# Attention, experts and FFN on one core: how the bias stage feeds the first head pair

## What is computed

```
scores = scale * np.matmul(q, k.transpose(0, 1, 3, 2))
psi_rel = np.log1p(np.abs(rel))
psi_i = np.log1p(np.maximum(pos[:, None].astype(np.float32), 1.0))
x = (psi_rel / psi_i)[..., None]
h = np.maximum(x @ w1 + b1, 0.0)
bias = h @ w2
scores = scores + bias.transpose(2, 0, 1)[None, :, :, :]
```

## Time and profile before

| | us |
|---|---|
| median of 3 runs | 1107.94 |
| lowest and highest | 1107.51, 1108.87 |
| profiled execution, its own time | 1108.25 |
| its span in the profile | 1106.4 |
| bias stage in it: first hidden tile to last store issued | 8.3 to 64.4 |
| TensorE busy over the span | 1060.3 (96%) |
| VectorE busy | 742.5 (67%) |
| ScalarE busy | 484.6 (44%) |
| GpSimd busy | 202.9 (18%) |

### The profile page before, as it was taken

One profiled execution on the slowest core, in us unless ns is written; L12 is line 12 of the kernel. 1 busy time (PEld: TensorE's weight loads), 2 busy tenths in 40 slices (PEclk: granted clock), 3 DMA queues, 4 the chain that ended last, 5 costly groups with the idle time before them and its releaser, 6 DMA issues.

```text
span 1106.4 us, 23091 instructions
## 1 busy us (share of the span) xinstructions
PE 1060.3 (96%) x7160; PEld 937.0 (85%) x7161; DVE 742.5 (67%) x1249; ACT 484.6 (44%) x972; POOL 202.9 (18%) x196
## 2 busy tenths in 40 slices
PE   5889999999999989999999999999999999999996
PEld 2367777777776889999999989999999999999995
DVE  8965555565655745775646479977777777777764
ACT  6987767677776343654444243221211212112111
POOL 2035525252540231221212000010010100100101
PEclk9999999999999989999999999999999999999998
DMA  4973643735531581773523180020000100100000
GB/s 138 293 227 83 179 111 84 204 82 118 168 69 33 176 292 52 201 201 50 201 50 88 59 257 1 22 58 0 28 28 0 57 0 0 57 0 0 29 1 29
DMA packets 87126, 103.11 MB, mean 93 GB/s; under 512 B 49536, under 2 KB 60800, under 8 KB 87088
## 3 DMA queue, kind: packets, MB, share of 16 engines
q1 hardware_dynamic: 83056, 89.27, 28.9%
q0 software_dynamic: 4032, 13.37, 4.3%
HBM read 77.25 MB, written 25.37 MB: 93 GB/s over the span
## 4 chain that ended last, share of the span: by engine, by line
PE 86%; DVE 5%; issue 3%; DMA 2%; ACT 2%; POOL 1%; SPq 0%; DVEq 0%; ACTq 0%; POOLq 0%
PE psum L1721 25%; PE psum L1737 12%; PE psum L1237 10%; PE psum L1246 10%; PE psum L443 8%; PE psum L562 7%; PE psum L547 6%; PE psum L267 3%; PE psum L575 2%; DVE f_eg L1676 1%; PE psum L1223 1%; DMA bias_ihj<-b_res 1%; DMA f_vraw<-fv 1%; ACT a_pr L672 0%; PE psum L1282 0%
## 5 line engine op out<-in xcount | busy, mean ns | idle before, releaser
L1676 DVE RECIPROCAL f_eg<-f_eg 128x384 f32<-128x384 f32 x72 | 183.2, 2545 | 0.0
L1643 ACT ACTIVATE f_eg<-psum 128x384 f32<-128x384 f32 x72 | 35.4, 492 | 330.9 <-PE psum L1721 330.9
L611 DVE CUSTOM_DVE_ANT_0 a_sc<-psum,a_bias 128x576 f32<-128x576 f32 x144 | 108.1, 753 | 79.9 <-PE psum L443 60.2
L1721 PE MATMUL psum<-f_x,f_ghi 128*128 (+1 forms) x576 | 147.8, 337 | 2.3 <-DVE f_eg L1680 1.1
L1721 PE MATMUL psum<-f_x,f_vhi 128*128 (+1 forms) x576 | 146.1, 334 | 0.0
L672 ACT ACTIVATE a_pr<-a_sc,a_nmax 128x576 f32<-128x576 f32 x144 | 111.6, 775 | 39.3 <-DVE a_nmax L611 32.8
L1721 PEld LDWEIGHTS psum<-f_x,f_ghi 128*128 128x128 f32 x576 | 105.7, 188 | 9.2 <-issue 2.6
L547 PE MATMUL psum<-ident,a_pr 128*128 128x128 f32 x720 | 102.5, 273 | 2.3 <-ACT a_pr L672 1.6
L1721 PEld LDWEIGHTS psum<-f_x,f_vhi 128*128 128x128 f32 x576 | 104.0, 188 | 0.0
L443 PE MATMUL psum<-a_khi,a_qs 128*128 128x288 f32 x320 | 102.5, 337 | 1.0 <-DVE a_nmax L611 0.7
L1611 POOL DMA_INDIRECT out<-f_ob,f_cols x18 | 17.5, 974 | 466.8 <-ACT f_ob L1629 463.5
(11 more groups left out here) (240 smaller groups left out, 2355.8 us busy)
## 6 DMA issues: line engine op xcount, KB each, us to landing
e_raw<-ew SPq DMA_DIRECT2D x16, 1024.0 KB, 9.7
bias_ihj<-b_res SPq DMA_DIRECT2D x36, 288.0 KB, 2.8
a_qraw<-q SPq DMA_DIRECT2D x32, 288.0 KB, 5.3
a_kraw<-k SPq DMA_DIRECT2D x32, 288.0 KB, 5.8
a_bias<-bias_ihj SPq DMA_DIRECT2D x16, 576.0 KB, 6.9
xn_t<-e_yn SPq DMA_DIRECT2D x8, 576.0 KB
a_v<-v SPq DMA_DIRECT2D x32, 128.0 KB, 2.4
x_tokens<-a_xp SPq DMA_DIRECT2D x64, 64.0 KB, 1.7
```

The lines of the kernel that those rows point to most:

```text
L611: e.tensor_tensor_reduce(sc[:, h, :].rearrange("p (a s) -> p a s", a=2), s_ps[:, h, :, 0:HALF], bias[:, 2 * s + h, :].rearrange("p (c s) - ...
L1643: e.activation(self.eg[:, k % 2, :], self.g_ps[k % 2][:, 0:CHUNK], ACT.Exp, scale=-1.0).then_inc(self.s_e, 1)
L1676: e.reciprocal(x, x).then_inc(self.s_c, 1)
L1721: mm = e.matmul(acc[:, 0:CHUNK], a, b, start=(q == 0 and i == 0), stop=(q == KD - 1 and i == 2))
```

## The change

Bias tiles are loaded one head at a time, in 288 KB with packets of 2304 bytes, after steps 11, 12, 19, 20, 27, 28 and, for the fourth tile, behind the store of step 35. v of the first pair is loaded after steps 13 to 16, q and k of the second pair in four transfers after steps 21 to 24, the gate weights after steps 0 and 1. In the later pairs a bias tile is also loaded as two transfers. GpSimd no longer casts the first pair; VectorE does, behind its last hidden tile: cast and subtraction of k, eviction of step 33, cast and subtraction of q, eviction of step 35. ScalarE leaves these two evictions out and loads the exponential's table behind the eviction of step 34. TensorE and the stores wait for VectorE's evictions by a semaphore of their own.

```diff
@@ -107,7 +107,8 @@
     CT = S + OFF
     CUT = 508
     PER = NS // 4
-    TILES = {10: 0, 18: 1, 26: 2, 34: 3}
+    TILES = {11: (0, 0), 12: (0, 1), 19: (1, 0), 20: (1, 1), 27: (2, 0), 28: (2, 1), 35: (3, 0)}
+    SHARED = (NS - 3, NS - 1)
     place = arena.run(arena.FRONT)
     table = place("b_table", [P, CT])
     dist_i = place("b_dist_i", [P, CT], i32)
@@ -131,7 +132,7 @@
     upper, lower = slice(CUT, CT), slice(0, CUT)
     s_id, s_z, s_w, s_io, s_go, s_d, s_ln, s_tab, s_low = (
         sem("b_" + n) for n in ("id", "z", "w", "io", "go", "d", "ln", "tab", "low"))
-    s_hp, s_hv, s_mm, s_ev = sem("b_hp"), sem("b_hv"), sem.loop("b_mm"), sem.loop("b_ev")
+    s_hp, s_hv, s_mm, s_ev, s_evd = sem("b_hp"), sem("b_hv"), sem.loop("b_mm"), sem.loop("b_ev"), sem("b_evd")
     s_st = [sem.loop(f"b_st{u}") for u in range(4)]
 
     def hidden(e, s, par, r4, done):
@@ -146,8 +147,10 @@
 
         def store(it, u):
             s = it * 4 + u
-            e.wait_ge(s_ev, sem.at(s_ev, s + 1))
-            sem.apart(e, s + 1)
+            if s in SHARED:
+                e.wait_ge(s_evd, sem.at(s_evd, SHARED.index(s) + 1))
+            else:
+                e.wait_ge(s_ev, sem.at(s_ev, s + 1 - sum(x < s for x in SHARED)))
             e.dma_start(biasd[bass.ds(s * P, P), :], res[:, u, :]).then_inc(s_st[u], 16)
 
         def landed(steps):
@@ -156,11 +159,14 @@
         for s in range(NS):
             store(s // 4, s % 4)
             if s in TILES:
-                landed(8 * TILES[s] + 8)
-                more["bias tile"](e, TILES[s])
+                t, h = TILES[s]
+                if h == 0:
+                    landed(8 * t + 8)
+                more["bias tile"](e, t, (h,))
             more["loads"](e, s)
+        more["bias tile"](e, 3, (1,))
         landed(NS)
-        more["bias tile"](e, 4)
+        more["bias tile"](e, 4, (0, 1))
 
     def gpsimd(e):
         e.memset(warm[:, :], 0.0).then_inc(s_z, 1)
@@ -216,7 +222,16 @@
         with e.Fori(1, PER) as it:
             for u in range(4):
                 step(it, u)
-        more["VectorE"](e)
+
+        def evict(s):
+            u = s % 4
+            e.wait_ge(s_mm, sem.at(s_mm, s + 1))
+            e.wait_ge(s_st[u], sem.at(s_st[u], s // 4 * 16))
+            e.tensor_scalar(res[:, u, :].rearrange("p (a b) -> p a b", a=2), acc[:, u, :, 0:HALF],
+                            invp[:, s:s + 1], None, ALU.mult).then_inc(s_evd, 1)
+        for i, s in enumerate(SHARED):
+            more["VectorE"](e, i)
+            evict(s)
 
     def scalar(e):
         e.wait_ge(s_z, sem.at(s_z, 1))
@@ -239,6 +254,8 @@
             e.wait_ge(s_mm, sem.at(s_mm, s))
             if following:
                 hidden0(s + 3, (u + 3) % 4)
+            if not following and s in SHARED:
+                return
             e.wait_ge(s_mm, sem.at(s_mm, s + 1))
             e.wait_ge(s_st[u], sem.at(s_st[u], it * 16))
             e.activation(res[:, u, :].rearrange("p (a b) -> p a b", a=2), acc[:, u, :, 0:HALF], ACT.Copy,
@@ -250,9 +267,8 @@
             for u in range(4):
                 step(it, u, True)
         for u in range(4):
-            if u == 3:
-                more["ScalarE"](e)
             step(PER - 1, u, u == 0)
+        more["ScalarE"](e)
 
     def tensor(e):
         e.wait_ge(s_w, sem.at(s_w, 16))
@@ -267,9 +283,10 @@
                         mm = e.matmul(acc[32 * r4:32 * r4 + 32, u, half, 0:HALF], w2d,
                                       hid[:, u, r4, half * HALF:(half + 1) * HALF], start=True, stop=True)
                 mm.then_inc(s_mm, 1)
-        for h in range(2):
-            e.wait_ge(s_ev, sem.at(s_ev, NS - 3 + h))
-            more["TensorE"](e, h)
+        e.wait_ge(s_ev, sem.at(s_ev, NS - 3))
+        more["TensorE"](e, 0)
+        e.wait_ge(s_evd, sem.at(s_evd, 1))
+        more["TensorE"](e, 1)
     return sync, tensor, scalar, vector, gpsimd
 
 
@@ -310,12 +327,18 @@
         sem.loop("a_" + n) for n in ("s", "b", "e", "t", "o", "oe", "bk", "r", "x"))
     s_kept = [sem.loop(f"a_t{g}") for g in range(3)]
 
-    def load_qk(e, pair, u, halves=(0, 1)):
-        for half in (slice(64 * i, 64 * i + 64) for i in halves):
+    def load_half(e, pair, u, i, of_k):
+        half = slice(64 * i, 64 * i + 64)
+        if of_k:
+            e.dma_start(kraw[half, u, :], kt[bass.ds(pair, 1), :, :].rearrange("a p s -> p (a s)")).then_inc(s_k[u], 16)
+        else:
             e.dma_start(qraw[half, u, :, :].rearrange("p a s -> p (a s)"),
                         qt[bass.ds(pair, 1), :, :, :].rearrange("a p h s -> p (a h s)")).then_inc(s_q[u], 16)
-            e.dma_start(kraw[half, u, :], kt[bass.ds(pair, 1), :, :].rearrange("a p s -> p (a s)"))\
-                .then_inc(s_k[u], 16)
+
+    def load_qk(e, pair, u):
+        for i in range(2):
+            for of_k in range(2):
+                load_half(e, pair, u, i, of_k)
 
     def load_v(e, pair, u, parts=range(4)):
         va, vb = (v[bass.ds(pair % B * H + pair // B * 2 + h, 1), :, :] for h in range(2))
@@ -326,14 +349,16 @@
         for i in parts:
             e.dma_start(*cuts[i]).then_inc(s_v[u], 16)
 
-    def load_bias(e, hp, s):
+    def load_bias(e, hp, s, heads=(0, 1)):
 
         if s == MIX:
-            for a in range(2):
+            for a in heads:
                 e.dma_start(bias[64 * a:64 * a + 64, 2 * s, :], biasd[BLK:S, bass.ds(hp * 2 + a, 1), :]
                             .rearrange("i a j -> i (a j)")).then_inc(s_bias[s], 16)
         else:
-            e.dma_start(bias[:, 2 * s:2 * s + 2, :], biasd[s * P:s * P + P, bass.ds(hp * 2, 2), :]).then_inc(s_bias[s], 16)
+            for h in heads:
+                e.dma_start(bias[:, 2 * s + h, :], biasd[s * P:s * P + P, bass.ds(hp * 2 + h, 1), :]
+                            .rearrange("i a j -> i (a j)")).then_inc(s_bias[s], 16)
 
     def set_constants(e):
         for u in range(2):
@@ -344,18 +369,21 @@
             e.tensor_copy(xw[:, :, h, 0:64], ident[:, 64 * h:64 * h + 64].unsqueeze(1).to_broadcast([P, H // 2, 64]))\
                 .then_inc(s_init, 1)
         e.wait_ge(s_init, sem.at(s_init, 5))
+
+    def first_split(e, part):
+
+        if part:
+            low = both(0, slice(64, P))
+            e.wait_ge(s_q[0], sem.at(s_q[0], 32))
+            e.wait_ge(s_init, sem.at(s_init, 2))
+            e.tensor_copy(both(0, slice(0, P)), qraw[:, 0, :, :]).then_inc(s_qh, 1)
+            e.wait_ge(s_qh, sem.at(s_qh, 1))
+            e.tensor_tensor(low, qraw[64:P, 0, :, :], low.bitcast(f32), ALU.subtract).then_inc(s_low, 1)
+            return
         e.wait_ge(s_k[0], sem.at(s_k[0], 32))
         e.tensor_copy(khi[:, 0, :], kraw[:, 0, :]).then_inc(s_sp, 1)
-        e.wait_ge(s_q[0], sem.at(s_q[0], 32))
-        e.tensor_copy(both(0, slice(0, P)), qraw[:, 0, :, :]).then_inc(s_qh, 1)
-
-    def first_low(e):
-
-        low = both(0, slice(64, P))
         e.wait_ge(s_sp, sem.at(s_sp, 1))
         e.tensor_tensor(klo[:, 0, :], kraw[:, 0, :], khi[:, 0, :].bitcast(f32), ALU.subtract).then_inc(s_low, 1)
-        e.wait_ge(s_qh, sem.at(s_qh, 1))
-        e.tensor_tensor(low, qraw[64:P, 0, :, :], low.bitcast(f32), ALU.subtract).then_inc(s_low, 1)
 
     def split_k(e, it, u):
 
@@ -391,17 +419,17 @@
 
     def loads(e, step):
 
+        if step in (0, 1):
+            if step == 0:
+                e.wait_ge(s_init, sem.at(s_init, 3))
+            e.dma_start(xw[64 * step:64 * step + 64, :, step, 64:XW],
+                        wg.rearrange("(p h d) e -> h d p e", h=2, d=64)[step]).then_inc(s_wg, 16)
         if step in (2, 4, 6, 8):
             small(e, step // 2 - 1)
-        if step in (12, 14, 16, 20):
-            if step == 12:
-                e.wait_ge(s_init, sem.at(s_init, 3))
-            load_v(e, 0, 0, ((12, 14, 16, 20).index(step),))
-        if step in (22, 24):
-            load_qk(e, 1, 1, (step // 2 - 11,))
-        if step in (28, 30):
-            h = step // 2 - 14
-            e.dma_start(xw[64 * h:64 * h + 64, :, h, 64:XW], wg.rearrange("(p h d) e -> h d p e", h=2, d=64)[h]).then_inc(s_wg, 16)
+        if step in (13, 14, 15, 16):
+            load_v(e, 0, 0, (step - 13,))
+        if step in (21, 22, 23, 24):
+            load_half(e, 1, 1, (step - 21) // 2, (step - 21) % 2)
 
     def split_done(e, p):
 
@@ -606,7 +634,7 @@
             unit = p * TPP + 2 * s + h
             e.wait_ge(s_s, sem.at(s_s, unit + 1))
             e.wait_ge(s_e, sem.at(s_e, unit if s == 0 and h == 0 else unit - 2 if s == 0 else unit - 1))
-            e.wait_ge(s_bias[s], sem.at(s_bias[s], (p // B + 1) * (32 if s == MIX else 16)))
+            e.wait_ge(s_bias[s], sem.at(s_bias[s], (p // B + 1) * 32))
             sem.apart(e, p)
             e.tensor_tensor_reduce(sc[:, h, :].rearrange("p (a s) -> p a s", a=2), s_ps[:, h, :, 0:HALF],
                                    bias[:, 2 * s + h, :].rearrange("p (c s) -> p c s", c=2),
@@ -724,7 +752,7 @@
 
```

(2 more changed lines are left out.)

## The result

The changed kernel takes 1109.78 us (median of 20 runs, 1107.45 to 1112.36) where the kernel before takes 1107.47 in the same comparison (20 runs, 1105.81 to 1111.34): ratio 1.0021, 95% interval 1.0013 to 1.0028. The forecast was 1106.4, range 1105.0 to 1108.7. The profiled execution has an own time of 1110.77 us and a span of 1108.9, against 1108.25 and 1106.4.

A forecast was written before the change was run, and what follows sets the result against it. TensorE holds 86% of the chain, so only an earlier start of the first pair, where ScalarE is late, was to count: 1108.25 - 1.5 = 1106.75, less 0.3 as that execution lay above the median, 1106.4; range 1105.0 to 1108.7.

The forecast's parts named there:

- GpSimd's casts go: Bias stage: without GpSimd's casts VectorE's hidden tiles aren't stretched, and the last ends 1.78 us earlier, at 55.43.
- What VectorE gets in their place: VectorE behind its last hidden tile: two casts at 0.87 us, two subtractions, two evictions at 0.75, ending at 61.11.
- The eviction of step 33 waits for a store: VectorE's eviction of step 33 waits for step 29's store, landing at 57.7, and starts at 57.8: costs 0.3 us.
- rival D: First pair: all cover holds, no store wait and a short cast; gain 1.8 to 2.0 us, 1105.7; chance 0.13.
- Rival A: VectorE's casts run at one column a cycle, 1.36 us instead of 0.87; costs 1.0 us, 1107.4; chance 0.10.
- B: Step 33's eviction waits for a store landing at 59.9; first exponential at 64.7, 0.75 us slower, 1108.7; chance 0.12.
- The gain at the first exponential: ScalarE's first exponential of the first pair comes at 62.47 instead of 63.96 us, a gain of 1.5 us.
- Moves that cost nothing: Moved loads and extra transfers, also in later pairs, are covered; SyncE pays some 0.4 us each, no tile is late.
- All later stages hang on the first pair and shift with it: Behind the first pair: every later stage moves earlier by the same 1.5 us gained at the first exponential.
- Rival C: First pair's start isn't what binds; later tiles or next pairs' v and q take the gain back, 1107.9; chance 0.10.
- slower: Whole kernel measured above 1110.2 us, from the tail of the case where step 33's eviction waits long; chance 0.04.

The follow-up runs named there:

- engines_only: Kernel before with only the casts and two evictions moved to VectorE and the table load behind step 34's eviction; loads as before: ratio 1.0002.
- loads_only: Kernel before with only the loads spread and cut by head; casts stay on GpSimd, evictions on ScalarE: ratio 1.0019.
- before_own_tokens: Kernel before with the experts' token-list stores on a semaphore of their own: ratio 1.0005 to the kernel before.
- before_plus_16: Kernel before plus 16 small loads that nothing reads, issued by SyncE near 103 us: ratio 1.0030.
- before_own_tokens_2: Repeat on another chip of the kernel before with the token-list stores on their own semaphore: ratio 1.0021.
- after_whole_own_tokens: Changed kernel with the later pairs' bias tiles whole again and the token-list stores on their own semaphore: ratio 1.0007 to the kernel before.

## Why the prediction was wrong

**"GpSimd's casts go": right.** No hidden tile is stretched any more (0.52 to 0.55 us each); the last ends at 55.45, forecast 55.43.

**"What VectorE gets in their place": right, with the cast a little dear.** 0.79 and 0.75 us where 0.87 was taken. The estimate of 0.76 worked out from the Trainium skill's page (VectorE: DVE Perf Modes, The perf-mode tier table) agrees with the second. The eviction from PSUM took 0.81 and 0.82 instead of 0.75.

**"The eviction of step 33 waits for a store": right in kind, too small.** In the first profile of the changed kernel it started at 57.43, at once, as in rival D, and the first exponential stood at 62.24, forecast 62.5. That was luck: the other six changed fronts waited 0.35 to 1.22 us, so the wait is 0.7 in the mean of seven where 0.3 was taken. Rival A is out, and so is B's wait of 2.5 us.

**The gain at the first exponential: 0.5 us in the mean, where 1.5 was forecast.** The first two profiles differ by 1.72, but the earlier trace rows has the exponential 0.2 later than the mean of its kernel, and the changed one's first profile has it 1.0 earlier than the mean of its own. And what is gained doesn't outlast the pair. TensorE's pause before the first scores, 2.3 to 3.4 us in the seven changed fronts, and the half clock behind it were not in the working. From the first transposes to the routing's first matmul an unchanged front takes 299.6 us (ten of eleven profiles), a changed one 299.9 to 300.7. engines_only, which has the row of work on VectorE but not the spread loads, has a pause of 1.56 us, full clock and 299.6; loads_only has half clock and 300.4. So this loss comes with the loads' part, and not with the row on VectorE alone. At the routing the changed front stands at 364.70 in the mean of seven, the unchanged one at 364.30 in the mean of eleven: the front's gain is nil or a small loss.

**The step that failed for the sign** is in "Moves that cost nothing": "In later pairs four extra transfers in each of three reloads cost SyncE some 0.4 us each; a tile has 1 us and more to spare". That priced the transfers by the engine that issues them and by the tile that waits. Both were right: no later tile was late. But together with the four of the first pair they changed when other transfers of the same queue land, 580 us on, at a place that has no slack: TensorE's pause there was 0.51 us already, and 0.38 us stays when nothing waits for the lists (before_own_tokens). The price, by the first two profiles, is 2.7 us of pause plus 1.5 of half clock, less what the front was ahead. In the second profile of the changed kernel the pause was 2.70 us and the clock stayed full, so the 1.5 isn't paid every time. **"All later stages hang on the first pair and shift with it"** failed at the same place: the shift of the start was found at 76 us and, 0.3 larger, at 630, and not at 642. Rival C (the start of the pair isn't what binds) came nearest, but its bound of 1107.9 took it that a gain could at most be taken back; nothing in the list of rivals could lose more than a store's lateness in the first pair, which is why slower had only 0.04.

**What is settled and what is open.** Settled: the loss is in the loads' part (1.0019 alone); it is a matter of the queue and not of what is loaded (before_plus_16, 1.0030); it needs the wait for the queue at the boundary: once the lists aren't waited for, changed and unchanged are level in the mean of two jobs (1.0012 and 1.0013), and with the value weights moved as well, again (0.9994 and 0.9994). That the second wait is what kept the 0.1% in between is argued from the profiles; the ratios scatter too much to show it. The Trainium skill (DMA: Bandwidth & Descriptors, Queues, rings and completion order) has each DMA's semaphore increment land only behind every earlier write of the same DMA engine. The value weights of before_own_tokens_2, issued behind the lists, don't contradict that, but they land 5.1 us behind the lists, so it isn't what set their time; no run here isolates it. Open: why 16 transfers more delay the last lists by 2 us and 12 don't, whether the count of packets or of transfers matters, and why some pauses of TensorE have half clock behind them and others not. Each profile is one execution, and the first pause scatters by half a microsecond between executions of one kernel, the second by more than one.

## What to carry to other kernels

Extra transfers aren't free because their issue is covered: look for every place further on where an engine waits for the same queue with less than some 2 us to spare (the landing moved by about 2 here), above all at a stage's end, and price it. Small scattered stores (lists of 4-byte items) can take long to land, 7.4 to 10.5 us here: look for what waits for them together with other data. Taking one of the two waits away moved the pause by 10 us and returned nothing; with both away the changed kernel was level with the kernel before, and a gain isn't shown. And before a gain is read against one profile, look how much that point scatters: here 2.7 us for a change forecast to bring 1.5.

## What was unexpected of the hardware

16 unread loads of 512 bytes, 0.008 MB in all, slow an 1108 us kernel by 0.30% when issued at some 103 us; what the profile shows of it is a landing 2 us later at 641 us, with the pause and the half clock behind it. Three transfers of 4-byte packets, 1.1 KB in all, take 7.4 to 10.5 us from issue to landing, with the DMA engines nearly idle for most of it (the DMA view of the kernel before has 0 to 6 GB/s from 633 to 638 us, the lists being issued by 632.5 and landed by 639.9). And half clock follows some pauses of TensorE and not others. At the boundary it stood behind those of 3.08, 3.22 and 3.33 us and not behind one of 2.70; at the second pause behind 1.86 and 2.04 us and not behind one of 2.55 (after_whole_own_tokens). In the changed kernel's first profile it cost 1.5 us on top of a pause of 3.22.
